# Attention, SoLU block and hard-swish block on one core: the second expert block as two sweeps of Strassen products, its activations in device memory between them

## The chip, the cores and the metric

One core of a Trainium2 chip. The time is that of the device in microseconds (us), median over runs; less is better.

## The reference

Chunked attention over 768 positions (4 batches, 8 heads, chunks of 32 with 16 before and 8 behind, and 8 memory rows), then two expert blocks over its 3072 tokens of 512 channels. The change touches the second:

```
def _moe_ref(x, w_in, w_out, g_ln):       # 3072x512, 512x1024, 1024x512
    h = x @ w_in
    ...
    solu = h * softmax(h)
    ...
    return (layer_norm(solu) * g_ln) @ w_out

def _moe2_ref(x, w_in, w_out):            # 3072x512, 512x2048, 2048x512
    h = x @ w_in
    relu6 = np.clip(h + 3.0, 0.0, 6.0)
    g = h * relu6 / 6.0
    return g @ w_out
```

All is float32. The kernel writes every operand of a large product as a high part in float32r (a cast) and a low part (operand less high part), and forms a product in three passes: high by high, high by low, low by high.

## The kernel before

The engines are programmed one by one, in the order in which the code stands; semaphores tie them together. `batch(b)` runs attention and the first expert block together, over eight steps `kk` per batch; `work` says which pieces fall into a step. `batch(B, last=True)` is the last one, with what is left: `turn_ln` (transposes of the normalised tile), `hidden` (first product) and `project` (second product, 24 matmuls of 384 tokens in each of four steps), whose result ACT copies in `store_x2` to `x2_out` and stores to device memory, `x2_scratch`. POOL's `normalise` makes the normalised tile.

The second block (`group`, six groups of 512 tokens) has all its weights in SBUF (`w2`, high and low). For each of 16 chunks of 128 hidden channels PE forms the hidden product (`hidden2`, through `split_products`, L505): 4 chunks of K by 3 passes, 12 matmuls of 512 tokens. ACT takes relu(h+3) (L753), DVE the minimum with 6 and the product with h (L896), ACT the high part (L763), DVE the low part (`low`, L783). Then `output` (L613): 4 token tiles by 3 passes, 12 matmuls of 512 output channels with `g_t` as weights. That is 6 x 16 x 12 = 1152 matmuls of each kind. Hidden products run two chunks ahead of output products. ACT's `copy_out` scales and copies the result (L745), SP stores it.

The weights of the second block come in 16 pieces: POOL issues two DMAs for each (L332, L337), ACT casts the high part (`high_weights`, L699), DVE subtracts the low part (`low_weights`). Five of them and the first tokens (`high_x2`, L687) fall into the last batch, where ACT and DVE have time, and so does the first hidden product, between the last transposes and the last four projections:

```
                    if w["mm2_3"]:
                        project(i, 3, ii, last and ii)
                    if last and kk == TPG:
                        hidden2(0, 0, 0, True)
```

## Time and profile before

| | |
|---|---|
| median of 3 runs | 984.63 us (984.3 to 985.13) |
| span of the profiled execution | 984.4 us |
| PE busy | 953.5 us, 97%, 5480 matmuls |
| weight loads of PE | 810.9 us, 82% |
| DVE / ACT / POOL busy | 484.9 / 410.6 / 101.3 us |
| bytes from and to device memory | 41.95 MB read, 12.58 MB written |
| mean granted clock of PE | 0.990 |

The profiled execution is given by its span, from its first to its last instruction; it lies 0.2 us under the median of the runs. PE means matmuls, PEld its weight loads, and a matmul's duration contains a pipeline's depth: the distance from one start to the next is its cost in a stream, not its duration. A busy share is an average over the whole program.

### The profile page before, as it was taken

The numbers are of one execution on the slowest core, as the hardware profiler recorded it, in microseconds if no ns is written. First come the engines' busy times: TensorE is split into PE (matmuls) and PEld (weight loads), VectorE is DVE, ScalarE is ACT, GpSimd is POOL, SyncE is SP. The second block draws the span as 40 slices with busy tenths as digits, with TensorE's granted clock in tenths as the row PEclk, the third lists the DMA queues.
The fourth block names the chain that finished last, engine by engine and source line by source line (L and its number), as shares of the span: only waits on it lengthen the run. The fifth ranks groups of instructions, "written<-read, shape, count | busy, mean of one in ns | idle before, by whom it ended". The sixth has DMA issues, their size and how long they took to land.

```text
span 984.4 us, 14941 instructions
## 1 busy us (share of the span) xinstructions
PE 953.5 (97%) x5480; PEld 810.9 (82%) x5480; DVE 484.9 (49%) x849; ACT 410.6 (42%) x1058; POOL 101.3 (10%) x138
## 2 busy tenths in 40 slices
PE   7788999999999999999999999999999999999998
PEld 6667888888888888899888888888878888888887
DVE  5787777777777767673652232223223322322221
ACT  5455565656555555543542322222223222323222
POOL 6363101001010101012310000000000000000000
PEclk9987999999999999999999999999999999999999
DMA  9533333332323432024430101001010101001001
GB/s 208 127 79 76 76 76 75 76 67 64 78 52 75 74 75 56 28 72 152 154 107 1 43 1 43 21 23 43 0 45 1 43 1 43 0 1 44 1 1 43
DMA packets 107304, 55.22 MB, mean 56 GB/s; under 512 B 93944, under 2 KB 98040, under 8 KB 107256
## 3 DMA queue, kind: packets, MB, share of 16 engines
q1 hardware_dynamic: 98904, 35.66, 16.0%
q0 software_dynamic: 3744, 12.59, 4.1%
q10 hardware_dynamic: 4608, 6.29, 1.8%
q8 instruction: 34, 0.56, 0.2%
q14 instruction: 14, 0.11, 0.0%
HBM read 41.95 MB, written 12.58 MB: 55 GB/s over the span
## 4 chain that ended last, share of the span: by engine, by line
PE 91%; DVE 5%; ACT 2%; issue 1%; DMA 1%; SPq 0%; DVEq 0%
PE banks L505 52%; PE banks L613 27%; PE banks L459 3%; PE banks L496 2%; PE banks L485 2%; PE banks L472 2%; PE banks L428 2%; DVE prob L807 1%; DMA k_in<-in_k_dram 1%; ACT prob L663 1%; DVE small L803 1%; PE banks L520 1%; DVE small L796 0%; DVE score L791 0%; DVE small L841 0%
## 5 line engine op out<-in xcount | busy, mean ns | idle before, releaser
L505 PE MATMUL banks<-x,w 128*128 128x512 f32 x1152 | 276.8, 389 | 0.7 <-issue 0.7
L613 PE MATMUL banks<-w,g_t 128*128 128x512 f32 x1152 | 276.4, 389 | 0.0
L505 PEld LDWEIGHTS banks<-x,w 128*128 128x128 f32 x1152 | 216.2, 188 | 45.7 <-issue 0.9
L613 PEld LDWEIGHTS banks<-w,g_t 128*128 128x128 f32 x1152 | 216.2, 188 | 45.1 <-DVE g_t L783 0.2
L896 DVE SCALAR_TENSOR_TENSOR g_raw<-g_raw,banks 128x512 f32<-128x512 f32 x96 | 66.1, 688 | 279.2 <-ACT g_raw L753 279.2
L753 ACT ACTIVATE g_raw<-banks,small 128x512 f32<-128x512 f32 x96 | 66.2, 690 | 275.0 <-PE banks L505 275.0
L505 PE MATMUL banks<-y_t,w_out 128*128 128x384 f32 x768 | 140.3, 337 | 0.0
L505 PE MATMUL banks<-w_in,x_t 128*128 128x512 f32 x552 | 133.7, 398 | 1.1 <-DVE solu L837 1.1
L505 PEld LDWEIGHTS banks<-y_t,w_out 128*128 128x128 f32 x768 | 132.1, 188 | 0.4
L505 PEld LDWEIGHTS banks<-w_in,x_t 128*128 128x128 f32 x552 | 103.5, 191 | 23.2 <-DVE solu L837 1.4
L663 ACT ACTIVATE prob<-score,small 96x128 f32<-96x128 f32 x256 | 99.2, 392 | 15.8 <-DVE small L796 15.8
L783 DVE TENSOR_TENSOR g_t<-g_raw,g_t 128x512 fp32r<-128x512 f32 x96 | 66.5, 693 | 70.5 <-ACT g_t L763 70.5
L763 ACT CAST g_t<-g_raw 128x512 fp32r<-128x512 f32 x96 | 59.7, 622 | 79.6 <-DVE g_raw L896 79.6
L791 DVE SCALAR_TENSOR_TENSOR score<-banks,mask 96x512 f32<-96x512 f32 x64 | 43.6, 681 | 27.0 <-PE banks L459 27.0
L807 DVE TENSOR_TENSOR prob<-prob,small 96x512 f32<-96x512 f32 x64 | 52.8, 825 | 2.2
L663 ACT ACTIVATION_READ_ACCUMULATOR prob<-score,small 96x1 f32 x256 | 48.7, 190 | 0.0
L392 POOL TENSOR_TENSOR small<-small 128x1 f32<-128x1 f32 x24 | 13.2, 552 | 339.7 <-DVE small L849 339.7
L796 DVE TENSOR_REDUCE small<-score 96x4 f32<-96x512 f32 x64 | 43.7, 682 | 2.2
L680 ACT COPY x_out<-banks 128x384 f32<-128x384 f32 x32 | 15.4, 480 | 67.8 <-PE banks L505 67.8
L669 ACT CAST x_t<-banks 128x384 fp32r<-128x384 f32 x32 | 15.3, 478 | 63.8 <-PE banks L485 63.8
L472 PE MATMUL banks<-ident,prob 96*128 96x96 f32 x256 | 30.5, 255 | 9.8 <-DVE prob L807 8.2
L459 PE MATMUL banks<-k_t,q_t 64*96 64x128 f32 x512 | 37.3, 287 | 1.1 <-ACT k_t L643 0.7
(61 smaller groups left out, 742.6 us busy)
## 6 DMA issues: line engine op xcount, KB each, us to landing
q_in<-in_q_dram SPq DMA_DIRECT2D x32, 192.0 KB, 3.7
x_scratch<-x_out ACTq DMA_DIRECT2D x32, 192.0 KB, 1.9
x_raw<-x_scratch SPq DMA_DIRECT2D x6, 1024.0 KB, 5.2
out_dram<-o_stage SPq DMA_DIRECT2D x24, 256.0 KB, 2.2
...
w_raw<-in_moe_w_in_dram POOLq DMA_DIRECT2D x16, 256.0 KB, 3.4
w_raw<-in_moe_w_out_dram POOLq DMA_DIRECT2D x16, 256.0 KB, 3.3
```

The lines of the kernel that those rows point to most:

```text
L459: mm = pe.matmul(score_ps[:, place(h), :], q_t[r, h // 2, :], k_t[r, h // 2, :], start=True, stop=True, skip_group_check=True)
L472: mm = pe.transpose(turn_ps[half][:, x * TQ:(x + 1) * TQ], prob[:, HB * half + x, :], ident[0:TQ, 0:TQ])
L505: mm = pe.matmul(psum, stationary(a, kc), moving(m, kc), start=(x == 0), stop=(x == len(passes) - 1))
L613: mm = pe.matmul(out_ps[t], g_t[:, c % 4, a, t * P:(t + 1) * P], w2[:, c, m, KD * P:PIECE], start=(c == 0 and x == 0), stop=(c == KF2 - 1 ...
L663: last = nc.scalar.activation(prob[:, h, :], score[:, h, :], ACT.Exp, bias=smax[:, h:h + 1], accum_out=ssum[:, h:h + 1])
L753: nc.scalar.activation(g_raw[:, c % 2, :], h2_ps[c % 4], ACT.Relu, bias=three).then_inc(relu_done, 1)
L763: nc.scalar.copy(g_t[:, c % 4, HI, :], g_raw[:, c % 2, :]).then_inc(g_hi_done, 1)
L783: return nc.vector.tensor_tensor(dst, src, hi.bitcast(F32), ALU.subtract)
L791: nc.vector.scalar_tensor_tensor(out=score[:, hs, :], in0=score_ps[:, hs, :], scalar=SCALE, in1=mask[:, kind, :].unsqueeze(1).broadcast_to ...
L796: nc.vector.tensor_reduce(smax[:, hs], score[:, hs, :], AX_X, ALU.max, negate=True).then_inc(smax_done, 1)
L807: nc.vector.tensor_tensor(prob[:, hs, :], prob[:, hs, :], srec[:, hs].unsqueeze(2).broadcast_to([TQ, HB, NK]), ALU.mult).then_inc(prob_don ...
L896: nc.vector.scalar_tensor_tensor(out=g_raw[:, c % 2, :], in0=g_raw[:, c % 2, :], scalar=6.0, in1=h2_ps[c % 4], op0=ALU.min, op1=ALU.mult). ...
```

## The change

Both products of the second block are split into 2 x 2 blocks and formed by Strassen's method in Winograd's form: seven products of blocks in place of eight, with four combinations of blocks on either operand ahead and seven additions behind. This needs all hidden channels before the second product, so there are two sweeps:

- First sweep: eight pairs `p` (hidden channel tiles p and p+8) by three units `g` of 1024 tokens. A unit is seven products of 2 chunks of K by 3 passes, 6 matmuls of 512 tokens each. POOL combines the weights (`mix_ws`) and subtracts their low parts (`low_ws`), ACT casts (`high_ws`). POOL combines x once (`mix_x`), ACT casts it (`high_xs`), DVE subtracts (`low_xs`); x stays in SBUF. ACT keeps partial sums (`keep`) and takes the relu (`relu_of`), DVE adds (`sum_of`) and gates (`gate`), SP stores the gated activations to `g_scratch` in device memory.
- Second sweep: six groups of 512 tokens by eight pairs `p`. SP loads four blocks of activations (`load_gs`), DVE combines (`mix_gs`, four operations of 256 columns), ACT casts 7 x 256 = 1792 columns (`high_gs`), DVE subtracts as many (`low_gs`), PE multiplies: 7 products x 2 x 3 = 42 matmuls of 256 columns. In the first group `mix_vs`, `high_vs` and `low_vs` (on POOL for odd, on DVE for even pairs) prepare the output weights. At a group's end ACT keeps the first product and DVE adds the others (`finish`).

The preparation of x and of the first weights goes into the last batch; `hidden2(0, 0)`, `high_x2` and `high_weights` are gone from it. The core of the diff:

```diff
@@ SP @@
+            load_ws(0)
+            sp.wait_ge(h_done, NG * MPG)
...
+            load_x(0)
+            sp.wait_ge(x2_done, KD * (NG - 1))
...
+            load_x(1)
+            sp.wait_ge(x2_done, KD * NG)
             for s in range(2):
                 sp.wait_ge(x2_free[s], 16 * (1 + 2 * NG))
-            load_x2(1)
...
+            load_x(2)
+            pair(0, first=True)
+            with sp.Fori(1, PAIRS - 1) as p:
+                pair(p)
+            pair(PAIRS - 1, last=True)
+            store_g(PAIRS - 1, 2, 12)
+            sp.wait_ge(prod_done[3], 3 * PAIRS)
+            for p in range(3, PAIRS):
+                load_vs(p)
@@ POOL @@
+            mix_ws(0)
+            low_ws(0)
+            mix_x(0)
+            mix_x(1)
+            mix_x(2)
+            mix_ws(1)
+            low_ws(1)
+            with pool.Fori(2, PAIRS) as p:
+                mix_ws(p)
+                low_ws(p)
+            for p in range(PAIRS):
+                mix_vs(p)
+                if p >= 2 and p % 2 == 0:
+                    low_vs(p - 1)
+            low_vs(PAIRS - 1)
@@ PE @@
-                    if last and kk == TPG:
-                        hidden2(0, 0, 0, True)
...
+            def product(i, g, ps, fresh):
+                passes = [(kc, a, m) for kc in range(2) for a, m in ((HI, HI), (HI, LO), (LO, HI))]
+                for x, (kc, a, m) in enumerate(passes):
+                    mm = pe.matmul(ps, ws[:, a, W_OF[i], kc, :], xs[g][X_OF[i]][:, m, kc, :],
+                                   start=(fresh and x == 0), stop=(x == len(passes) - 1), skip_group_check=True)
+                mm.then_inc(prod_done[i], 1)
...
+            def unit(p, g, first):
...
+                product(1, g, acc_ps[g], True)
+                if g > 0:
+                    third(p, g - 1, first)
...
+                pe.wait_ge(part_kept, 3 * u + 1)
+                product(6, g, acc_ps[g], False)
...
+                product(2, g, two_ps[g], True)
+                operands(7, p, g, first)
+                pe.wait_ge(part_kept, 3 * u + 2)
+                product(7, g, acc_ps[g], False)
...
+            def group(grp, first=False):
+                for p in range(PAIRS):
+                    pe.wait_ge(gs_lo_done, PAIRS * grp + p + 1)
...
+                    for i in M_ORDER:
+                        mm = mix_product(i, grp, p, first)
@@ ACT @@
                     if last and kk == 3:
-                        high_weights(0)
+                        act.wait_ge(wt_done, 4)
+                        high_ws(0, ORDER)
...
-                    if last and kk > 3:
-                        high_weights(kk - 3)
+                    if last and kk == 4:
+                        for n in range(7):
+                            high_xs(0, n)
+                    if last and kk in (5, 6):
+                        for n in range(4 * (kk - 5), 4 * (kk - 5) + 4 - (kk == 6)):
+                            high_xs(1, n)
...
+            for s in range(2):
+                act.wait_ge(x2_free[s], 16 * (1 + 2 * NG))
+            unit(0, 0, first=True)
+            high_xs(2, 0)
+            high_xs(2, 1)
+            unit(0, 1, first=True, then=[lambda n=n: high_xs(2, n) for n in range(2, 7)])
...
+            def group(grp, first=False, last=False):
+                for p in range(PAIRS):
+                    if first and p + 1 < PAIRS:
+                        high_vs(p + 1)
+                    if p + 2 < PAIRS:
+                        high_gs(grp, p + 2)
+                    elif not last:
+                        high_gs(grp + 1, p + 2 - PAIRS)
@@ DVE @@
+            def mix_gs(grp, p):
+                n = PAIRS * grp + p
+                x = p % 4
+                dve.wait_ge(g_here[x], 16 * (2 * grp + p // 4 + 1))
+                for k, (to, a, b, op) in enumerate(((4, 1, 3, ALU.add), (1, 0, 1, ALU.subtract),
+                                                    (5, 4, 0, ALU.subtract), (6, 2, 5, ALU.subtract))):
+                    if k:
+                        dve.wait_ge(gt_done, 4 * n + k)
+                    nc.vector.tensor_tensor(gs_raw[x][:, to, :], gs_raw[x][:, a, :], gs_raw[x][:, b, :], op
+                                            ).then_inc(gt_done, 1)
+
+            def low_gs(grp, p):
+                x = p % 4
+                dve.wait_ge(gs_hi_done, PAIRS * grp + p + 1)
+                low(gs[x][:, LO, :, :], gs_raw[x][:, :, :], gs[x][:, HI, :, :]).then_inc(gs_lo_done, 1)
...
+            def group(grp, first=False, last=False):
+                for p in range(PAIRS):
+                    if p + 2 < PAIRS:
+                        low_gs(grp, p + 2)
+                    elif not last:
+                        low_gs(grp + 1, p + 2 - PAIRS)
+                    if first and p + 1 < PAIRS and (p + 1) % 2 == 0:
+                        low_vs(p + 1)
+                    if p + 3 < PAIRS:
+                        mix_gs(grp, p + 3)
+                    elif not last:
+                        mix_gs(grp + 1, p + 3 - PAIRS)
+                finish(grp, first)
```

How the order moves, at three places. ACT in the last batch, before, from the last but one cast of a normalised tile (`y_t`) on; `x_out` is the copy of a projection, `w` a piece of weights:

```order
244 L656 CAST y_t_52<-banks 128x4x128 [waits y_turned] x2
245 L699 CAST w_69<-w_raw 128x1024 [waits w_raw_here0,h_done]
246 L680 COPY x_out<-banks 128x384 [waits x2_free1,x2_done]
247 L682 DMA x_scratch<-x_out 128x384 [waits x2_copied]
248 L656 CAST y_t_52<-banks 128x4x128 [waits y_turned] x2
249 L699 CAST w_69<-w_raw 128x1024 [waits w_raw_here1]
250 L680 COPY x_out<-banks 128x384 [waits x2_free0,x2_done]
251 L682 DMA x_scratch<-x_out 128x384 [waits x2_copied]
252 L699 CAST w_69<-w_raw 128x1024 [waits w_raw_here0]
253 L680 COPY x_out<-banks 128x384 [waits x2_free1,x2_done]
254 L682 DMA x_scratch<-x_out 128x384 [waits x2_copied]
255 L699 CAST w_69<-w_raw 128x1024 [waits w_raw_here1]
```

The same place now; `ws` are weights of the second block, `xs` its tokens:

```order
243 L885 CAST y_t_52<-banks 128x4x128 [waits y_turned] x2
244 L917 CAST ws<-ws_raw 128x256 [waits wt_done]
245 L917 CAST ws<-ws_raw 128x256 x6
246 L909 COPY x_out<-banks 128x384 [waits x2_free1,x2_done]
247 L911 DMA x_scratch<-x_out 128x384 [waits x2_copied]
248 L885 CAST y_t_52<-banks 128x4x128 [waits y_turned] x2
249 L926 CAST xs_0_70<-xs_raw_0_91 128x1024 [waits x_here0]
...
255 L926 CAST xs_2_72<-xs_raw_2_93 128x1024 [waits x_here0]
256 L909 COPY x_out<-banks 128x384 [waits x2_free0,x2_done]
257 L911 DMA x_scratch<-x_out 128x384 [waits x2_copied]
```

Between two copies of `x_out` stood one cast of a weight piece; now seven casts stand there, most of them with a wait for POOL's combinations (`xt_done`). What POOL does for them, behind its last normalisation (`ln`):

```order
98 L522 TENSOR_SCALAR ln<-solu,small 128x1024 [waits rstd_done,mask_ready]
99 L552 TENSOR_TENSOR ws_raw<-ws_raw 128x256 [waits ws_here]
100 L552 TENSOR_TENSOR ws_raw<-ws_raw 128x256 [waits wt_done] x3
101 L558 TENSOR_TENSOR ws<-ws_raw,ws 128x256 [waits ws_hi_done] x7
102 L567 TENSOR_TENSOR xs_raw_4_95<-xs_raw_6_97,xs_raw_0_91 128x1024 [waits x_here0]
```

Before, POOL issued weight DMAs at this place. DVE inside the loop of the second sweep, two steps of it (`gs` activations with high and low part, `gs_raw` as loaded and combined):

```order
497 L1088 TENSOR_TENSOR gs_125<-gs_raw_129,gs_125 128x1792 [waits gs_hi_done]
498 L1241 ISA
499 L1246 TENSOR_TENSOR gs_raw_126<-gs_raw_126 128x256 [waits g_here0]
500 L1245 ISA
501 L1246 TENSOR_TENSOR gs_raw_126<-gs_raw_126 128x256 [waits gt_done]
502 L1245 REGISTER_ALU
503 L1246 TENSOR_TENSOR gs_raw_126<-gs_raw_126 128x256 [waits gt_done]
504 L1245 REGISTER_ALU
505 L1246 TENSOR_TENSOR gs_raw_126<-gs_raw_126 128x256 [waits gt_done]
506 L1251 REGISTER_ALU
507 L1088 TENSOR_TENSOR gs_122<-gs_raw_126,gs_122 128x1792 [waits gs_hi_done]
508 L1246 TENSOR_TENSOR gs_raw_127<-gs_raw_127 128x256 [waits g_here1]
```

Before, the loop had an operation of 512 columns with a wait for `relu_done` and one with a wait for `g_hi_done`, 96 times; now four of 256 columns stand between two of 1792, each behind the one before it.

## Rows read from the trace of the kernel before

**Rows 1.** The page: busy time by engine, and the chain that ended last by engine
```profile
PE 953.5 (97%) x5480; PEld 810.9 (82%) x5480; DVE 484.9 (49%) x849; ACT 410.6 (42%) x1058; POOL 101.3 (10%) x138
...
PE 91%; DVE 5%; ACT 2%; issue 1%; DMA 1%; SPq 0%; DVEq 0%
```

**Rows 2.** By window: span; PE, PEld, DVE, ACT, POOL busy (count); PEclk, DMA, GB/s
```profile
25.00:34.00 9.00, 4.71 (x53) 3.80 (x52) 8.39 (x12) 4.59 (x20) 7.12 (x7) 1.00 0.88 193
34.10:37.30 3.20, 2.96 (x10) 2.48 (x11) 3.13 (x6) 1.98 (x9) 0.00 (x0) 0.50 0.46 169
...
760.00:980.00 220.00, 220.00 (x973) 182.21 (x972) 58.87 (x86) 60.23 (x96) 0.00 (x0) 1.00 0.04 15
```

**Rows 3.** Timeline of PE, 440 to 466: start, us, line, operation, shapes, count
```profile
440.22 1.03 PE L496 MATMUL banks<-ident,ln 128*128 128x128 f32 x8
441.01 2.99 PE L505 MATMUL banks<-x,w 128*128 128x512 f32 x12
443.84 16.83 PE L505 MATMUL banks<-y_t,w_out 128*128 128x384 f32 x96
460.51 5.64 PE L505 MATMUL banks<-x,w 128*128 128x512 f32 x24
```

**Rows 4.** DVE by line and shape: total busy, mean ns of one | idle before
```profile
L783 DVE TENSOR_TENSOR g_t<-g_raw,g_t 128x512 fp32r<-128x512 f32 x96 | 66.5, 693 | 70.5 <-ACT g_t L763 70.5
L896 DVE SCALAR_TENSOR_TENSOR g_raw<-g_raw,banks 128x512 f32<-128x512 f32 x96 | 66.1, 688 | 279.2 <-ACT g_raw L753 279.2
...
L783 DVE TENSOR_TENSOR w<-w_raw,w 128x1024 fp32r<-128x1024 f32 x16 | 20.4, 1272 | 20.5 <-ACT w L699 20.3
```

**Rows 5.** ACT by line and shape
```profile
L753 ACT ACTIVATE g_raw<-banks,small 128x512 f32<-128x512 f32 x96 | 66.2, 690 | 275.0 <-PE banks L505 275.0
L763 ACT CAST g_t<-g_raw 128x512 fp32r<-128x512 f32 x96 | 59.7, 622 | 79.6 <-DVE g_raw L896 79.6
...
L699 ACT CAST w<-w_raw 128x1024 fp32r<-128x1024 f32 x16 | 16.8, 1049 | 3.0 <-DMA w_raw<-in_moe_w_out_dram 1.8 <-ACT x_out L680 1.2
```

**Rows 6.** POOL by line and shape
```profile
L395 POOL TENSOR_SCALAR ln<-solu,small 128x1024 f32<-128x1024 f32 x24 | 28.8, 1200 | 4.3 <-POOL small L392 4.3
...
L358 POOL TENSOR_TENSOR w_out<-w_raw,w_out 128x1024 fp32r<-128x1024 f32 x4 | 9.7, 2433 | 0.3
...
L352 POOL TENSOR_SCALAR w_raw<-w_raw,small 128x512 f32<-128x512 f32 x8 | 5.4, 686 | 0.9 <-DMA w_raw<-in_moe_w_out_dram 0.9
```

**Rows 7.** DMA issues, the page's part 6
```profile
x_raw<-x_scratch SPq DMA_DIRECT2D x6, 1024.0 KB, 5.2
out_dram<-o_stage SPq DMA_DIRECT2D x24, 256.0 KB, 2.2
```

**Rows 8.** Weight loads of PE by line
```profile
L613 PEld LDWEIGHTS banks<-w,g_t 128*128 128x128 f32 x1152 | 216.2, 188 | 45.1 <-DVE g_t L783 0.2
```

**Rows 9.** Timelines of POOL (one row) and DVE (two rows), 30 to 34
```profile
30.39 2.34 POOL L358 TENSOR_TENSOR w_out<-w_raw,w_out 128x1024 fp32r<-128x1024 f32 x1
...
30.56 2.72 DVE L807 TENSOR_TENSOR prob<-prob,small 96x512 f32<-96x512 f32 x1
...
33.60 0.69 DVE L807 TENSOR_TENSOR prob<-prob,small 96x512 f32<-96x512 f32 x1
```

**Rows 10.** Timelines of ACT (two rows), DVE, POOL, 438 to 443
```profile
440.42 0.48 ACT L680 COPY x_out<-banks 128x384 f32<-128x384 f32 x1 [2.15 <-PE banks L505]
...
441.31 1.08 ACT L656 CAST y_t<-banks 128x512 fp32r<-128x512 f32 x2 [0.41 <-PE banks L496]
...
441.93 1.29 DVE L783 TENSOR_TENSOR y_t<-banks,y_t 128x512 fp32r<-128x512 f32 x2 [1.63 <-ACT y_t L656]
...
438.03 1.21 POOL L395 TENSOR_SCALAR ln<-solu,small 128x1024 f32<-128x1024 f32 x1 [0.18 <-POOL small L392]
```

**Rows 11.** Timelines of PE and of SP's queue at the end
```profile
972.92 8.32 PE L613 MATMUL banks<-w,g_t 128*128 128x512 f32 x36
...
979.86 2.37 SPq L296 DMA_DIRECT2D out_dram<-o_stage  x4
```

634 lines of the change are left out of this document (453 added, 181 removed).

## Prediction

> **What bounds the kernel now.** I read the page's busy times and its chain of waits first [rows 1]: TensorE (PE) is busy for 97% of the span, and 91% of the chain that ended last is PE. So time is won by fewer PE columns, as long as nobody else comes to set the pace. Next the stretches by window [rows 2]: in the 220 us from 760 on, PE issues 973 matmuls of 512 columns, one per 226.1 ns, at the full clock, while DVE is busy 27% and ACT 27%. The timeline of PE [rows 3] gives the other width: 96 matmuls of 384 columns between 443.84 and 460.51, one per 173.6 ns. Last the groups by shape for DVE, ACT and POOL [rows 4 to 6], since the change hands them much more.
>
> **Products, first sweep.** Eight products become seven at the same 512 columns: 8 x 3 x 7 x 6 = 1008 matmuls in place of 1152, that is 144 x 226.7 ns (226.1 rounded up for loop ends) = **32.6 us saved**. One unit (seven products of six matmuls) is 9.5 us. DVE has per unit seven operations of 0.69, 4.8 us, and ACT seven of 0.69 and a third of seven small casts, some 5.6 us [rows 4, 5]. Their chain also fits: product 3 of the unit before ends, DVE adds (0.69), ACT takes the relu (0.69) and keeps the partial sum (0.69 at most), 2.1 us with hand-offs, and product 7, which needs the last, starts 2.7 us after product 3 has ended. Stores of 256 KB take 2.2 us [rows 7] and have a whole unit. I cost this sweep at PE's own pace; if the casts of new weights fall into that chain, it loses some tenths in each of 16 units, at most 5 us.
>
> **Products, second sweep.** 6 x 8 x 7 x 6 = 2016 matmuls of 256 columns in place of 1152 of 512. No row has this form. A line through the two widths (0.41 ns per column) gives 121 ns; with 128 columns, transposes with the same 128-column weights follow each other at 0.79 us for 8, 99 ns [rows 3], so a weight load does not hold the stream above that there. From below I bound it at 113 (half of 226.1), from above at 188 ns, the length of one LDWEIGHTS [rows 8]. I take 121, the nearest in form: 42 matmuls, a pair of channel tiles, are **5.1 us**, the sweep 244 us, 17 under before, if PE sets the pace.
>
> **It does not: DVE and ACT do.** For each pair DVE forms four combinations of 256 columns, ACT casts 1792 columns, DVE subtracts 1792 columns. The program puts the subtraction for pair n directly behind the combinations of pair n and the combinations of n+1 behind it, so DVE stands idle during the cast, and the three times add up. DVE's tensor_tensor is 693 ns at 512 and 1272 at 1024 [rows 4], so 403 at 256 and 2140 at 1792; ACT's cast is 622 and 1049 [rows 5], so 1690 at 1792. 4 x 0.403 + 1.69 + 2.14 + 0.15 for hand-offs = **5.6 us per pair against PE's 5.1**. At the end of each group DVE adds seven products from PSUM at 0.69 (plus 0.03) = 5.0, behind which one cast (1.7) hides: 8 x 5.6 + 5.0 - 1.7 = **48.1 us per group** against 40.7 of PE. PE also waits at each group's start for the sums that free its banks, with gaps of some 4 us; it catches up within the group.
>
> **First group of that sweep.** DVE also subtracts three weight tiles (3 x 2.14), and POOL forms combinations and four subtractions. POOL's tensor_tensor takes 2.34 us at 1024, undisturbed [rows 9], 2.43 in the mean [rows 6]; with an intercept like that of its tensor_scalar (686 at 512, 1200 at 1024: 0.17) 0.72 at 256 and 4.0 at 1792. Five weight tiles are loaded only after the first sweep: 20 x 0.75 + 4 x 4.0 = 31 us. And POOL and DVE exclude each other: DVE's operation on prob from two SBUF operands starts at 30.56, inside POOL's from 30.39 to 32.73, and takes 2.72 in place of 0.69. I put the operations of ACT, DVE and POOL one behind the other, each engine in its order, POOL and DVE never at once. The subtractions of pairs 2 to 7 then end 9, 17, 31, 37, 51 and 56 us after the first sweep (two weight subtractions of 4.0 and 2.1 stand before every second one), those of the next group's pairs 0 and 1 at 67 and 73, the seven additions at 80, the next subtraction at **82**. With POOL free of charge the same list reads 7, 13, 20, 26, 34, 39, 47, 52, 59 and **61**. The Trainium skill, page "SBUF — State Buffer", section "Who interferes with whom", says that a DVE instruction with two SBUF inputs contends with a GpSimd one that reads SBUF, whoever came first holding the port. The trace agrees, with the 2.72 above; without that rule the first group would be 21 us shorter and the total 1016.
> After that four groups of 48.1 and five pairs of 5.6: 82 + 192.4 + 28 = 302.4, and PE's last pair with a lag of 2 us: **309.5 us from the end of the first sweep to PE's end**, where before had 1152 matmuls, 261.
>
> **Between the blocks.** Before, ACT's cast of a weight piece and 12 matmuls of the second block fill the last steps of the first block [rows 3, 10]. Now ACT casts seven pieces behind a wait for POOL's four combinations, and POOL comes to them only after its last normalisation, which ends at 439.24 [rows 10]. 439.3 + 3.2 = 442.5, casts 7 x 0.35 (0.41 by the same line, less what neighbours overlap) = 444.9, then the copy of x2 that stood at 440.42, and the cast of y_t, which began 0.9 us behind it and took 1.1: it now ends at 446.9, DVE's part 0.9 later, 447.8. PE has nothing after its transposes (440.22 and 0.8 to 0.9 us on, so 441.1): **6.7 us**. Four projections follow (4 x 4.2 = 16.8). The third needs the copy of the first, which in ACT's order stands behind seven casts that wait for POOL's combinations of x (4 x 2.4 at 1024 columns, some 10 us, and DVE's subtractions of 1.27 between them): first copy at 464 in place of 452, **8.5 us**. The fourth waits likewise for the next four casts: **6.2 us**. The first unit waits for ACT, which waits for the last store of x2: 2.3 us. The last third of x is loaded after that store: 2 MB, at 5.2 us per 1 MB [rows 7] 10.4 us, then POOL's combinations; meanwhile ACT stands before the casts in the second unit: 5.3 + 4.2 us. Sum **33.2 us**. After gaps the clock has fallen: at 34.10 to 37.30 it is 0.50 of full, the lower of the two levels, after a stretch in which PE was busy 4.71 of 9.00 us [rows 2], and 10 matmuls fill those 3.2 us; for five gaps I add 0 to 10, and take 4. **37 us** in all; what covers it, if POOL is quicker than I think, is nothing but its speed, so the range has 17 to 50.
> **Removed:** 16 casts and 16 subtractions of weights 24 of each for x, hidden behind PE now; POOL's 32 weight DMAs, hidden; both at nothing. What is added in DMA, 96 stores of 256 KB and 48 loads of 512 KB, is hidden as long as a load lands within the 10 us between its slot's release and its use.
>
> **The sum**, on the profiled execution (span 984.4; the median of runs is 984.63, 0.2 more): end of the first block 441.1 + 16.8 = 457.9; turn-over 37; first sweep 228.5; gives 723.4. Second sweep 309.5: 1032.9. Tail: before, PE ends at 981.24 and the last store at 984.4 [rows 11], 3.2; now an addition of 0.7 and a store of twice the size, 4.1. Total **1037 us**.
>
> **Rivals.** *PE sets the pace of the second sweep* (faster): if the cycle of combine, cast and subtract stays under 5.1 us, for which the wide operations would have to run 10% below the line through 512 and 1024 columns. Then 723.4 + 244 + 5 + 4 = 976, and about 950 with a light turn-over. For it stands only that DVE and ACT are at 27% now; against it the three durations. It decides at 5.1. *Weight loads bound the narrow matmuls* (slower still): 188 ns each, 2016 x 0.188 = 379, 723.4 + 379 + 8 = 1110. Against it the 99 ns of the transposes; for it, that those are another kind of matmul. The Trainium skill, "TensorE: Matmul & The Clock Gate", section "LDWEIGHTS (loading the stationary operand)", gives columns over 1.2, an estimate of 107 ns for 128 columns, by which the load would hide under 121; no run here shows that width. *POOL and DVE hardly collide and the turn-over is short*: 61 in place of 82 and 17 in place of 37: 996 to 1016; part of my range. *The gains and losses cancel*: total within 0.2%.
>
> **Chances.** The least difference that a measurement of this kernel tells from none is about 0.2%, 2 us. Forecast with its bounds (slower) 0.87; weight loads 0.05, slower too; PE's pace, faster, 0.06; cancelled 0.02. So slower 0.92, same 0.02, faster 0.06. Range: down by 20 for the first group, or by 20 for the turn-over, not both in full: 1003. Up by 13 for the turn-over, 10 for a cycle of 5.8 in place of 5.6 (44 times), 5 for the first sweep: 1065.
>
> **What would show it.** Right: granted clock lowered and gaps of PE between 441 and 510; units of 9.5 us after; DVE's 1792-column subtraction near 2.14 and ACT's cast near 1.69, taking turns; pairs at 5.6 and groups at 48; DVE operations of 4 us or more beside POOL in the first group. Wrong: matmuls of 256 columns above 130 ns apart; PE without idle time behind gs_lo_done; PE busy straight through 441 to 510.

## The result, and the profile after

The changed kernel took 1049.44 us (median of 4 runs, 1049.16 to 1051.67), the kernel before 984.46 beside it on the same chip (4 runs): ratio 1.0665, 95% interval 1.065 to 1.0681. The forecast of 1037 had the sign right, and the time lies in its range of 1003 to 1065. The profiled execution has a span of 1047.5 us, and the numbers below are set against that.

First the page of the changed kernel: busy time by engine; the chain that ended last, by engine; of the costliest groups those of the new block. They answer to [rows 1] and [rows 4, 5, 8].

```profile
PE 929.1 (89%) x6200; PEld 830.8 (79%) x6200; DVE 706.2 (67%) x1092; ACT 481.4 (46%) x1109; POOL 238.4 (23%) x242
...
PE 56%; DVE 19%; issue 8%; ACT 8%; POOL 5%; DMA 2%; SPq 1%; DVEq 0%; ACTq 0%; POOLq 0%
...
L841 PE MATMUL banks<-vs,gs 128*128 128x256 f32 x2016 | 260.3, 294 | 50.8 <-DVE vs L1088 21.8
L841 PEld LDWEIGHTS banks<-vs,gs 128*128 128x128 f32 x2016 | 257.7, 203 | 53.5 <-issue 39.6
L770 PE MATMUL banks<-xs,ws 128*128 128x512 f32 x1008 | 235.2, 395 | 18.5 <-ACT part L976 18.5
...
L1038 ACT CAST gs<-gs_raw 128x1792 fp32r<-128x1792 f32 x48 | 81.0, 1688 | 205.8 <-DVE gs_raw L1246 205.8
...
L1088 DVE TENSOR_TENSOR gs<-gs_raw,gs 128x1792 fp32r<-128x1792 f32 x48 | 101.3, 2110 | 75.9 <-ACT gs L1038 75.7
...
L1246 DVE TENSOR_TENSOR gs_raw<-gs_raw 128x256 f32<-128x256 f32 x192 | 90.9, 473 | 4.9
```

TensorE did less (929.1 us in place of 953.5) and the kernel took longer: PE's share of the chain went from 91% to 56%, and VectorE and ScalarE have 27% between them, where they had 7%. The idle time in the last columns says where: 50.8 us of PE in the second sweep and 18.5 in the first; and VectorE stood 75.7 us behind ScalarE's cast of the gates, while ScalarE stood 205.8 behind VectorE's combinations. These are two engines that wait for each other by turns.

Next the windows of the changed kernel (span; busy time and count of PE, PEld, DVE, ACT, POOL; PEclk; DMA; GB/s): a stretch between the blocks, the steady part of the first sweep, and 180 us of the second, beside [rows 2].

```profile
445.00:452.00 7.00, 5.31 (x17) 5.34 (x18) 3.95 (x3) 1.89 (x4) 6.84 (x6) 0.52 0.34 126
513.50:711.00 197.50, 197.49 (x870) 162.67 (x870) 101.58 (x146) 102.87 (x192) 59.16 (x72) 1.00 0.36 129
820.00:1000.00 180.00, 163.86 (x1298) 162.35 (x1296) 126.98 (x178) 54.29 (x35) 0.00 (x0) 0.94 0.35 111
```

The first sweep runs as forecast: 870 matmuls in 197.5 us, 227.0 ns each, no idle time. In the second, PE is idle 16 of 180 us while DVE is busy 71%. In the stretch behind a gap of 6.18 us the granted clock is about half (0.52), near the lower of the two levels, as in [rows 2].

The timeline of PE in the changed kernel (start, us, line, operation, count, idle time before) in its three troubled places: between the blocks, at the turn of the sweeps, and at the group starts.

```profile
446.69 10.88 PE L682 MATMUL banks<-y_t,w_out 128*128 128x384 f32 x48 [6.18 <-DVE y_t L1088]
461.88 6.02 PE L682 MATMUL banks<-y_t,w_out 128*128 128x384 f32 x24 [4.32 <-ACT x_out L909]
472.26 5.99 PE L682 MATMUL banks<-y_t,w_out 128*128 128x384 f32 x24 [4.36 <-ACT x_out L909]
...
513.51 8.68 PE L770 MATMUL banks<-xs,ws 128*128 128x512 f32 x37 [1.82 <-ACT part L976]
...
721.92 9.93 PE L770 MATMUL banks<-xs,ws 128*128 128x512 f32 x36 [10.69 <-ACT part L976]
731.69 5.20 PE L841 MATMUL banks<-vs,gs 128*128 128x256 f32 x42
746.99 7.51 PE L841 MATMUL banks<-vs,gs 128*128 128x256 f32 x42 [10.10 <-POOL vs L580]
758.93 11.82 PE L841 MATMUL banks<-vs,gs 128*128 128x256 f32 x84 [4.44 <-DVE vs L1088]
781.86 12.23 PE L841 MATMUL banks<-vs,gs 128*128 128x256 f32 x84 [11.11 <-DVE vs L1088]
800.31 12.34 PE L841 MATMUL banks<-vs,gs 128*128 128x256 f32 x90 [6.23 <-DVE vs L1088]
...
903.86 0.95 PE L841 MATMUL banks<-vs,gs 128*128 128x256 f32 x6 [1.68 <-ACT held L1077]
907.64 41.98 PE L841 MATMUL banks<-vs,gs 128*128 128x256 f32 x330 [2.83 <-DVE o_stage L1280]
```

With these rows the loss can be laid out. If PE had never waited, the changed kernel would read: end of the first block 457.3 (transposes end at 440.5, and 16.8 of projections), 1008 x 226.7 ns = 228.5, 2016 x 120.1 ns = 242.1, tail 4.7: **932.6 us**, 52 under the span before. It took 115 more:

| stretch | lost by PE, us | from |
|---|---|---|
| between the blocks, up to 513.51 | 33 | 513.51 less 102 matmuls of the block (23.1), less 457.3 |
| turn of the sweeps | 12.4 | gap 10.69, and 36 matmuls in 9.93 in place of 8.2 |
| first group of the second sweep | 39.7 | 80.1 (731.7 to 811.8, the start of the next group's first matmul) in place of 336 x 120.1 ns = 40.4 |
| its five other groups | 29.2 | 231.0 (811.8 to 1042.8) in place of 201.8 |

The cycle of the steady groups, in the timeline of VectorE and then of ScalarE of the changed kernel:

```profile
803.63 2.03 DVE L1088 TENSOR_TENSOR gs<-gs_raw,gs 128x1792 fp32r<-128x1792 f32 x1 [1.75 <-ACT gs L1038]
805.58 1.80 DVE L1246 TENSOR_TENSOR gs_raw<-gs_raw 128x256 f32<-128x256 f32 x4
809.13 2.03 DVE L1088 TENSOR_TENSOR gs<-gs_raw,gs 128x1792 fp32r<-128x1792 f32 x1 [1.76 <-ACT gs L1038]
```

```profile
807.41 1.69 ACT L1038 CAST gs<-gs_raw 128x1792 fp32r<-128x1792 f32 x1 [3.81 <-DVE gs_raw L1246]
```

Subtraction 2.03, combinations 1.80, idle 1.76 while ScalarE casts for 1.69: from 803.63 to 809.13 is 5.50 us. PE's six-by-seven matmuls need 5.04. Of 47.0 us per group VectorE spends seven such cycles and 8.5 us on the last one, which has the additions in it; in that time it waits for nothing but ScalarE's cast. PE runs six of the eight pairs of a group at 5.04 us each, has then caught up, and pays at the group's start: gaps of 1.7 and 2.8 us, and a stretch at half clock behind them (granted clock 0.50 from 907.6 to 911).

### The profile page after: what moved, and what is told of

Its sections match the earlier page's. It is cut to its first block, busy times and chain, and to the rows that moved or that the text cites. A ratio compares the mean times of both kernels' runs of the same rounds, so it can differ in the third digit from the quotient of the medians.

```text
span 1047.5 us, 17721 instructions
## 1 busy us (share of the span) xinstructions
PE 929.1 (89%) x6200; PEld 830.8 (79%) x6200; DVE 706.2 (67%) x1092; ACT 481.4 (46%) x1109; POOL 238.4 (23%) x242
## 4 chain that ended last, share of the span: by engine, by line
PE 56%; DVE 19%; issue 8%; ACT 8%; POOL 5%; DMA 2%; SPq 1%; DVEq 0%; ACTq 0%; POOLq 0%
PE banks L682 22%; PE banks L770 19%; DVE gs_raw L1246 7%; ACT gs L1038 6%; PE banks L841 4%; POOL xs_raw L567 3%; PE banks L636 3%; DVE gs L1088 3%; PE banks L662 2%; PE banks L673 2%; PE banks L649 2%; PE banks L605 2%; DVE vs L1088 2%; DVE held L1280 1%; DVE prob L1112 1%
## 5 line engine op out<-in xcount | busy, mean ns | idle before, releaser
L841 PE MATMUL banks<-vs,gs 128*128 128x256 f32 x2016 | 260.3, 294 | 50.8 <-DVE vs L1088 21.8
L841 PEld LDWEIGHTS banks<-vs,gs 128*128 128x128 f32 x2016 | 257.7, 203 | 53.5 <-issue 39.6
L770 PE MATMUL banks<-xs,ws 128*128 128x512 f32 x1008 | 235.2, 395 | 18.5 <-ACT part L976 18.5
L770 PEld LDWEIGHTS banks<-xs,ws 128*128 128x128 f32 x1008 | 191.4, 191 | 62.1 <-ACT part L976 11.1
L1038 ACT CAST gs<-gs_raw 128x1792 fp32r<-128x1792 f32 x48 | 81.0, 1688 | 205.8 <-DVE gs_raw L1246 205.8
L682 PE MATMUL banks<-y_t,w_out 128*128 128x384 f32 x768 | 146.4, 347 | 14.9 <-ACT x_out L909 8.7
L1088 DVE TENSOR_TENSOR gs<-gs_raw,gs 128x1792 fp32r<-128x1792 f32 x48 | 101.3, 2110 | 75.9 <-ACT gs L1038 75.7
L682 PEld LDWEIGHTS banks<-w_in,x_t 128*128 128x128 f32 x552 | 103.2, 190 | 23.1 <-DVE solu L1142 1.4
L992 ACT ACTIVATE relu<-part,small 128x512 f32<-128x512 f32 x72 | 52.2, 724 | 97.4 <-DVE part L1203 97.4
L1246 DVE TENSOR_TENSOR gs_raw<-gs_raw 128x256 f32<-128x256 f32 x192 | 90.9, 473 | 4.9
L1212 DVE SCALAR_TENSOR_TENSOR part<-relu,part 128x512 f32<-128x512 f32 x72 | 54.0, 750 | 52.8 <-ACT relu L992 52.8
L1203 DVE TENSOR_TENSOR part<-part,banks 128x512 f32<-128x512 f32 x72 | 49.5, 687 | 53.0 <-PE banks L770 52.8
L976 ACT COPY part<-banks 128x512 f32<-128x512 f32 x72 | 41.6, 578 | 15.9 <-PE banks L770 13.5
```

What stands on the lines that cost most here:

```text
L682: mm = pe.matmul(psum, stationary(a, kc), moving(m, kc), start=(x == 0), stop=(x == len(passes) - 1))
L770: mm = pe.matmul(ps, ws[:, a, W_OF[i], kc, :], xs[g][X_OF[i]][:, m, kc, :], start=(fresh and x == 0), stop=(x == len(passes) - 1), skip_gr ...
L841: mm = pe.matmul(m_ps[i][:, s, :], gs[x][:, a, G_OF[i], s * P:(s + 1) * P], vs[p][:, m, V_OF[i], :], start=(p == 0 and s == 0 and n == 0), ...
L992: nc.scalar.activation(relu[r][:, :], src, ACT.Relu, bias=three).then_inc(relu_done[kind], 1)
L1038: nc.scalar.copy(gs[p % 4][:, HI, :, :], gs_raw[p % 4][:, :, :]).then_inc(gs_hi_done, 1)
L1088: return nc.vector.tensor_tensor(dst, src, hi.bitcast(F32), ALU.subtract)
```

## The experiments

Each run is set beside the kernel before on its own chip (984.3 to 985.3 us in median), and beside the 1047.5 of span that the change has.

### dve_ahead: the combination ahead of the subtraction

```diff
                 for p in range(PAIRS):
+                    if p + 3 < PAIRS:
+                        mix_gs(grp, p + 3)
+                    elif not last:
+                        mix_gs(grp + 1, p + 3 - PAIRS)
                     if p + 2 < PAIRS:
                         low_gs(grp, p + 2)
...
-                    if p + 3 < PAIRS:
-                        mix_gs(grp, p + 3)
-                    elif not last:
-                        mix_gs(grp + 1, p + 3 - PAIRS)
```

> The same instructions, with DVE's combinations for pair p+3 ahead of its subtraction for pair p+2 (they stood behind it), all through the second sweep. Theory 1 (combinations, cast and subtraction follow each other in one cycle, because DVE waits through ACT's cast): the cast now runs beside DVE's next combinations, DVE needs 3.8 us per pair, PE's 42 matmuls at 120 ns set the pace with 5.04 us. At a group's end the additions still come late by some 4 us, so groups of about 44 in place of 47.8 us; with the first and the last group about 22 us less, 1027. Theory 2 (DVE's total work, or the landing of the activations from device memory, sets the pace): nothing changes, 1049, groups of 47.8.

Measured: 1042.76 us (1039.34 to 1044.95), ratio 1.0572 (1.0547 to 1.0597). The timeline of PE in this run at a group start, and that of VectorE ahead of it:

```profile
907.39 42.08 PE L841 MATMUL banks<-vs,gs 128*128 128x256 f32 x336 [2.67 <-DVE o_stage L1280]
```

```profile
903.00 1.80 DVE L1246 TENSOR_TENSOR gs_raw<-gs_raw 128x256 f32<-128x256 f32 x4 [1.11 <-DMA gs_raw<-g_scratch]
904.72 2.02 DVE L1088 TENSOR_TENSOR gs<-gs_raw,gs 128x1792 fp32r<-128x1792 f32 x1
```

The wait for the cast is gone, and VectorE waits for loads of gates instead, which start when PE has freed a slot: within a group PE sets the pace now. A group takes 45.0 us ((997.08 - 817.01) / 4, by PE's gaps) in place of 47.0. What is left is not the cycle but the group's end: a gap of 2.7 us, and matmuls at a lower clock behind it (granted clock 0.76 from 907 to 914). So the cause was right and its price a third of what I expected, 6.7 us in place of 22. The second sweep alone is 7.1 us shorter in the profiled executions (304.0 in place of 311.1).

### dve_ahead_sums: the sums one step earlier as well

On top of that, the last combination of a group moved behind `finish`, so that the sums stand ahead of it:

```diff
-                    elif not last:
+                    elif not last and p < PAIRS - 1:
                         mix_gs(grp + 1, p + 3 - PAIRS)
...
                 finish(grp, first)
+                if not last:
+                    mix_gs(grp + 1, 2)
```

> As dve_ahead, and at a group's end the seven additions come ahead of the combinations for pair 2 of the next group, whose activations land only when PE has used its buffer. Theory 1: PE's wait at the start of a group shrinks from about 4 us to about 1, groups of about 41.5 us, total about 1014. Theory 2: nothing changes against after (1049). A mixed case: the time of dve_ahead, if PE's wait at the group's start comes from the subtraction and not from the additions.

Measured: 1021.89 us (1020.19 to 1023.16), ratio 1.0366 (1.0348 to 1.0384). PE's timeline of this run:

```profile
897.94 40.57 PE L841 MATMUL banks<-vs,gs 128*128 128x256 f32 x336 [0.22 <-DVE held L1280]
938.69 40.58 PE L841 MATMUL banks<-vs,gs 128*128 128x256 f32 x336 [0.18 <-DVE held L1280]
```

A group takes 40.8 us, 4.2 less again, at PE's own pace. The five groups take 203.7 us in place of 231.0, so 27.3 of the 29.2 us that they lost come from the order of one engine's instructions. No operation became shorter and none was left out: in the second sweep VectorE's subtractions of gates last 2203 ns in the mean (2112 in the change) and its combinations 481 (475). The sums' move alone was not run, so how the two moves share the gain is known in this order only. The 256-column matmuls take 120.7 ns over a whole group, against 120.1 in an undisturbed stretch, with a weight load for each, so the loads hide under them.

### pool_write_only: does GpSimd's reading hold VectorE?

```diff
-                nc.gpsimd.tensor_tensor(vs[p][:, LO, :, :], vs_raw[p][:, :, :], vs[p][:, HI, :, :].bitcast(F32),
-                                        ALU.subtract).then_inc(vs_lo_odd, 1)
+                nc.gpsimd.memset(vs[p][:, LO, :, :].bitcast(F32), 0.0).then_inc(vs_lo_odd, 1)
```

> POOL's four subtractions of 1792 columns of output weights (low parts of odd pairs) become memsets of the same columns to zero: the low parts of the weights of pairs 1, 3, 5 and 7 are left out. POOL writes as much but reads nothing. Theory 1 (POOL and DVE exclude each other where both read SBUF): DVE's subtractions of 1792 columns that took 5.8 us beside POOL's take 2.0 beside a memset, the first group is some 8 to 12 us shorter, total about 1039. Theory 2 (any operation of POOL holds DVE off): those subtractions take about 2.0 plus the memset's length, 3.7 us, and the total is about 1043.

Measured: 1035.91 us (1034.66 to 1038.2), ratio 1.0514 (1.0491 to 1.0537). This kernel leaves the low parts of the odd pairs' weights out. The rows of the changed kernel, GpSimd's and then VectorE's:

```profile
775.63 4.21 POOL L580 TENSOR_TENSOR vs<-vs_raw,vs 128x1792 fp32r<-128x1792 f32 x1 [4.58 <-ACT vs L1042]
```

```profile
775.94 5.78 DVE L1088 TENSOR_TENSOR vs<-vs_raw,vs 128x1792 fp32r<-128x1792 f32 x1
```

and those of this run, in the same order:

```profile
768.78 1.59 POOL L580 MEMSET vs<- 128x1792 f32 x1 [5.02 <-ACT vs L1041]
```

```profile
769.11 2.02 DVE L1087 TENSOR_TENSOR vs<-vs_raw,vs 128x1792 fp32r<-128x1792 f32 x1
...
771.04 3.56 DVE L1245 TENSOR_TENSOR gs_raw<-gs_raw 128x256 f32<-128x256 f32 x4
```

Beside a subtraction of GpSimd that reads two SBUF operands, VectorE's row lasts 5.78 us, from 0.31 behind GpSimd's start to 1.88 behind its end: in length that is GpSimd's instruction waited out and then VectorE's own 2.02. Beside a GpSimd operation that writes as much and reads nothing, it lasts 2.02. GpSimd's combinations, which still read, go on stretching VectorE's (3.56 for four in place of 1.80). That is the rule which the prediction drew from the Trainium skill, page "SBUF — State Buffer", section "Who interferes with whom"; the same section excepts a GpSimd instruction that only writes, and this run shows that too. The time fell by 12.4 us in span and 13.5 in median. In the changed kernel three of VectorE's rows stand beside GpSimd's subtractions (5.78, 5.78 and 5.57 in place of 2.02), 11 us of stretch. Together with those beside GpSimd's combinations, VectorE's rows of the first group are 20.8 us longer than at 2.02 and 0.45 each, which is the size that the forecast gave to this collision (21). The total does not price the collision alone: GpSimd's own rows fell from 4 us or more to 1.59 as well, four times, and its next combinations start sooner for it.

### last_unit: preparation inside the last unit of the first sweep

```diff
-            high_vs(0)
-            high_gs(0, 0)
-            unit(last, 2)
+            unit(last, 2, then=[lambda: None, lambda: None, lambda: high_vs(0), lambda: None,
+                                lambda: high_gs(0, 0)])
...
-            low_vs(0)
             mix_gs(0, 0)
-            unit(last, 2, then=[lambda: mix_gs(0, 1), lambda: low_gs(0, 0)])
+            unit(last, 2, then=[lambda: mix_gs(0, 1), lambda: low_vs(0), lambda: None, lambda: low_gs(0, 0)])
```

> ACT's casts of the first output weights and the first activations, and DVE's subtraction of those weights, stand inside the last unit of the first sweep, ahead of which they stood; nothing else is changed. Theory 1 (PE's gap from 711 to 722 is ACT waiting for POOL's and DVE's preparation of the second sweep, in its queue ahead of the copy that PE needs): the gap goes, at most 3 us of it come back at the start of the second sweep, and a stretch at half clock goes too: about 1040. Theory 2 (the weights of the second sweep land late anyway, and PE waits for them then): the gap moves behind the last unit, total 1047 to 1049.

Measured: 1044.97 us (1042.44 to 1046.84), ratio 1.061 (1.0582 to 1.0637). ScalarE's timeline of the changed kernel, where the 10.69 comes from:

```profile
714.21 1.68 ACT L1042 CAST vs<-vs_raw 128x1792 fp32r<-128x1792 f32 x1 [4.96 <-POOL vs_raw L575]
719.70 1.69 ACT L1038 CAST gs<-gs_raw 128x1792 fp32r<-128x1792 f32 x1 [3.81 <-DVE gs_raw L1246]
721.29 0.58 ACT L976 COPY part<-banks 128x512 f32<-128x512 f32 x1
```

and PE's of this run:

```profile
717.74 7.35 PE L770 MATMUL banks<-xs,ws 128*128 128x512 f32 x24 [2.87 <-ACT part L976]
726.55 5.30 PE L841 MATMUL banks<-vs,gs 128*128 128x256 f32 x42 [1.46 <-DVE gs L1087]
740.69 4.61 PE L841 MATMUL banks<-vs,gs 128*128 128x256 f32 x20 [8.84 <-POOL vs L580]
```

and GpSimd's of this run:

```profile
728.25 8.36 POOL L575 TENSOR_TENSOR vs_raw<-vs_raw 128x256 f32<-128x256 f32 x8 [13.14 <-DMA vs_raw<-in_moe_w_out_dram]
```

ScalarE stood 4.96 us for GpSimd's combinations and 3.81 for VectorE's with a copy behind them that PE needed. With the casts behind that copy, the gap falls from 10.69 to 2.87, one of 1.46 appears ahead of the second sweep, and that sweep starts at 726.55, 5.1 us sooner. The run as a whole gained 4.5, half of the 9 expected: the place is shown, but not all of the gap goes. The first group behind it keeps its length (79.0 us in place of 80.1): GpSimd's combinations for pairs 1 and 2 start at 728.25 in place of 735.92, and PE still waits 8.84 us for the first of them.

### stores_first, x_on_dve, casts_between_stores: the way between the blocks

Three kernels on the 33 us ahead of 513.51. In the profiled executions of the change and of the four kernels so far, which have the same code up to there, that instant lies between 512.65 and 514.94, so differences under some 2 us say nothing. The first kernel puts the casts of `ws` behind those of y_t, all casts of the first third of `xs` behind the last store of x2, and those of the second third, with VectorE's subtractions, into the first unit:

```diff
-                    if last and kk == 3:
-                        act.wait_ge(wt_done, 4)
-                        high_ws(0, ORDER)
                     if last and kk == 4:
-                        for n in range(7):
-                            high_xs(0, n)
-                    if last and kk in (5, 6):
-                        for n in range(4 * (kk - 5), 4 * (kk - 5) + 4 - (kk == 6)):
-                            high_xs(1, n)
+                        act.wait_ge(wt_done, 4)
+                        high_ws(0, ORDER)
...
             act.wait_ge(three_ready, 1)
+            for n in range(7):
+                high_xs(0, n)
...
+            unit(0, 0, first=True, then=[lambda n=n: high_xs(1, n) for n in range(7)])
+            high_xs(1, 6)
```

> Turn-over between the blocks: ACT's seven casts of the first weights move behind the last casts of the normalised tile, and all casts of x behind the last copy of a projection, so that no copy stands behind a cast that waits for POOL; DVE's subtractions follow. Amounts of work are unchanged. Theory 1 (PE's gaps between 440 and 478 are ACT's queue: copies behind casts that wait for POOL's combinations): the gap of 6.2 us before the projections shrinks to about 1.7, those of 4.3 and 4.4 between them go, the last third of x is loaded some 18 us earlier, and the total falls by about 17 us to about 1032. Theory 2 (POOL's combinations are the bound of this stretch, wherever the casts stand): the gaps move to the first units, total about 1045.

Measured: 1048.42 us (1046.77 to 1050.2), ratio 1.0643 (1.0619 to 1.0668). PE's timeline of this run:

```profile
442.30 16.91 PE L682 MATMUL banks<-y_t,w_out 128*128 128x384 f32 x96 [2.11 <-DVE y_t L1085]
462.64 2.90 PE L770 MATMUL banks<-xs,ws 128*128 128x512 f32 x6 [3.43 <-DVE xs L1085]
...
483.11 7.11 PE L770 MATMUL banks<-xs,ws 128*128 128x512 f32 x18 [7.75 <-ACT part L970]
```

The four projections run without a gap, as expected: PE's first three gaps shrink from 14.9 us to 2.1. But PE is steady from 508.71, only 4.8 us sooner, and the total is not clear of the change's: a miss of 16 us. ScalarE's queue was where PE waited, but the work behind it bounded the stretch. VectorE's row of this run, and GpSimd's in the changed kernel:

```profile
461.27 18.93 DVE L1085 TENSOR_TENSOR xs<-xs_raw,xs 128x1024 fp32r<-128x1024 f32 x7 [19.12 <-ACT xs L926]
```

```profile
446.88 23.82 POOL L567 TENSOR_TENSOR xs_raw<-xs_raw,xs_raw 128x1024 f32<-128x1024 f32 x8
```

With the casts behind the stores VectorE stood idle for 19.12 us, and then its seven subtractions took 2.7 us each beside GpSimd's combinations, where one alone takes 1.22; PE's gaps of 3.43 and 7.75 stand behind them.

The second leaves ScalarE's order as the change has it and moves `mix_x` from GpSimd to VectorE, ahead of the subtractions that read it (its definition, on VectorE with the same four operations, is left out here):

```diff
-            mix_x(0)
-            mix_x(1)
-            mix_x(2)
...
                 i = ORDER[n]
+                if n == 0:
+                    mix_x(g)
```

> The twelve combinations of x (1024 columns each) move from POOL to DVE, directly ahead of DVE's subtractions for the same tokens; ACT's order is as in after. Theory 1 (they are slow on POOL, 2.35 us against 1.27, and POOL and DVE hold each other off): first copy behind the casts at about 455 in place of 461, second at about 467 in place of 472, all that follows about 6 us earlier and a combination time of 5 in place of 11 us for the last third: total about 1037. Theory 2 (ACT's order alone makes the gaps): 1045 or more.

Measured: 1041.92 us (1041.0 to 1047.61), ratio 1.0594 (1.0556 to 1.0631); PE is steady from 506.38, 7.1 sooner. The third has that, puts the casts of `ws` later as `stores_first` did, and spreads ScalarE's casts of x three by three between the stores of x2:

```diff
+                    if last and kk == 7:
+                        for n in range(3):
+                            high_xs(1, n)
...
                     if last and kk == 4:
-                        for n in range(7):
+                        act.wait_ge(wt_done, 4)
+                        high_ws(0, ORDER)
+                        high_xs(0, 0)
+                    if last and kk in (5, 6):
+                        for n in range(3 * (kk - 5) + 1, 3 * (kk - 5) + 4):
                             high_xs(0, n)
-                    if last and kk in (5, 6):
-                        for n in range(4 * (kk - 5), 4 * (kk - 5) + 4 - (kk == 6)):
-                            high_xs(1, n)
...
+            unit(0, 0, first=True, then=[lambda n=n: high_xs(1, n) for n in range(3, 7)])
```

> Both of the last two: combinations of x on DVE, and ACT's casts of x spread three by three between the copies of the projections, those of the second third partly inside the first unit. Theory 1: projections run without gaps from about 442 to 459, the first unit starts at about 460 in place of 478, total about 1024. If one of the two theories of the turn-over is wrong, it is no better than the better of the two runs alone.

Measured: 1039.97 us (1035.93 to 1042.06), ratio 1.0547 (1.0514 to 1.058); steady from 502.13, 11.4 sooner than in the change, 8.9 of which reach the second sweep. So two causes are there: GpSimd's combinations of x, and ScalarE's order. `x_on_dve` does not part GpSimd's slowness (2.34 us at this width [rows 9] where VectorE takes 1.22) from its collision with VectorE. The second cause shows in PE's steady start (4.3 us sooner again) and not in the total, where the two kernels' times overlap. Taking both away gives 11 of 33 us. What is left is work on VectorE (it is busy 19.0 of the 21 us from 480 to 501 in the kernel `all`) and, ahead of PE's first gap there, ScalarE's waits for VectorE's combinations (3.73) and for the last store of x2 to land (2.04).

### all, all_2, all_sp: can the change be made to pay?

`all` joins casts_between_stores, last_unit and dve_ahead_sums, and gives the four subtractions of output weights that GpSimd did to VectorE (PE's wait for them changes with it):

```diff
                 mix_vs(p)
-                if p >= 2 and p % 2 == 0:
-                    low_vs(p - 1)
-            low_vs(PAIRS - 1)
...
-                    if first and p + 1 < PAIRS and (p + 1) % 2 == 0:
+                    if first and p + 1 < PAIRS:
                         low_vs(p + 1)
```

> All changes together: casts between stores with x on DVE, the last unit's order, DVE's combinations ahead of its subtractions with the additions ahead of the next group's third combination, and POOL's four subtractions of output weights moved to DVE (2.0 in place of 4.0 us of a port that only one of them holds). If the gains of the parts add up (25, 4 to 6, 27 and about 7 us): 1049 - 65 = 984, the time of before. The first group of the second sweep keeps it from less: its combinations, casts and subtractions of output weights take DVE and POOL some 65 us where PE needs 40.

Measured: 995.22 us (994.68 to 995.96), ratio 1.0104 (1.0086 to 1.0123), 54 us under the change, 11 over the 984 of the expectation and still 1.0% over the kernel before. PE's timeline of this run:

```profile
483.45 4.56 PE L764 MATMUL banks<-xs,ws 128*128 128x512 f32 x12 [5.08 <-ACT part L969]
...
728.77 6.95 PE L835 MATMUL banks<-vs,gs 128*128 128x256 f32 x42 [10.05 <-DVE vs L1080]
739.52 6.72 PE L835 MATMUL banks<-vs,gs 128*128 128x256 f32 x42 [3.80 <-DVE vs L1080]
...
773.07 55.94 PE L835 MATMUL banks<-vs,gs 128*128 128x256 f32 x450 [4.85 <-DVE vs L1080]
```

What is left is the way between the blocks, 20.8 us (501.19 less 23.1 and 457.3), and the first group, 71.5 us in place of 40.4 (from 713.42 to the first matmul of the next group at 784.93). Two more kernels went for those gaps. `all_2` moves ScalarE's last store of x2 ahead of the casts of the second third of x, one cast behind a part copy (left out here), and three loads, two of weights and one of gates, ahead of the stores in the last unit:

```diff
-                    if last and kk == 7:
-                        for n in range(3):
-                            high_xs(1, n)
                     if w["mm2_3"]:
                         store_x2(i, 3, last and ii)
+                    if last and kk == 7:
+                        high_xs(1, 0)
...
+                    if last and g == 2:
+                        sp.wait_ge(prod_done[3], 3 * p + 2)
+                        load_vs(1)
+                        load_gs(0, 3)
+                        load_vs(2)
                     if not (first and g == 0):
                         store_g(*before_unit(p, g), 12)
...
-                    if last and g == 2:
-                        sp.wait_ge(prod_done[3], 3 * p + 2)
-                        load_gs(0, 3)
-                        load_vs(1)
-                        load_vs(2)
```

> The kernel of the run all, with three moves more. (1) ScalarE: the last copy of x_out and its store come ahead of the casts of the second projection, which go behind it and between the part copies of the unit (0, 0); the gap of 5.30 us at 466.45 in that run stood behind a store that was issued at 463.71, after a cast that waited for VectorE. Theory: the gap falls to some 2 us. (2) ScalarE: the second cast of the third projection stands behind the first part copy of the unit (0, 1), where it stood ahead of it and waited for VectorE; the gap of 5.08 at 483.45 falls to under 1. (3) SyncE: in the last unit of the first sweep the loads of the output weights of pairs 1 and 2 and of pair 3's gates are issued ahead of the stores of the gates, not behind the first two of them; GpSimd's combination at 715.38, which waited for that load, comes some 5 us earlier, and the gap of 10.05 at 728.77 falls by 3 to 5. Sum: 995.2 - 3.3 - 4.5 - 4 = 983 us, about the kernel before (985.0, ratio 0.998). Rival: the preparation is bound by the sums of VectorE's work, as in stores_first, and the gaps only move: 990 to 995. A reading over 990 speaks for the rival.

Measured: 997.93 us (997.4 to 998.54), ratio 1.0135 (1.0118 to 1.0152), above the rival's 990 to 995 too. Against `all` it is 2.7 us slower, on another chip, and the intervals of the two ratios touch: it gained nothing, and may have lost. The gap of 5.30 fell to 1.90 and came back as 6.83 at 488.05; the gap of 10.05 fell to 5.58 and the next one rose from 3.80 to 7.04, and the first group takes 73.0 us in place of 71.5. `all_sp` takes only the loads, and lets the five last weight tiles take turns with the gates (the loads in the last unit, moved as in `all_2`, are left out here, and so is the shift of the group's own loads to pair 7 and later):

```diff
             pair(PAIRS - 1, last=True)
+            sp.wait_ge(prod_done[3], 3 * PAIRS)
+            load_vs(3)
             store_g(PAIRS - 1, 2, 12)
-            sp.wait_ge(prod_done[3], 3 * PAIRS)
-            for p in range(3, PAIRS):
-                load_vs(p)
+            load_vs(4)
+            for p in range(4, PAIRS - 1):
+                sp.wait_ge(gs_used, p - 3)
+                load_gs(0, p)
+                load_vs(p + 1)
```

> The kernel of the run all with SyncE's loads around the turn of the sweeps in another order, and nothing of all_2's ScalarE moves. The output weights of pairs 1 and 2 are issued ahead of the stores in the last unit of the first sweep; the five last weight tiles, which stood as one block of 2.5 MB ahead of the gates of pair 4, now take turns with the gates of pairs 4 to 6. In all, VectorE waited 2.60, 0.30, 2.25 and 0.97 us for gates in the first group, and GpSimd's weights of pair 1 came at 715.38. Theory (late loads are the rest of the first group's loss beside VectorE's own work): the gap of 10.05 falls to about 5.6, as in all_2, and those four waits fall by about 4 in sum: 995.2 - 4.5 - 4 = 987 us, ratio 1.002. Rival (VectorE's work sets the first group, 5.9 us per pair against TensorE's 5.1, and loads that come earlier only move the gaps): 993 to 996, with VectorE busy nearly without idle time between 713 and 773.

Measured: 1000.5 us (998.53 to 1002.28), ratio 1.0157 (1.0142 to 1.0173). VectorE's timeline of this run:

```profile
758.04 1.80 DVE L1252 TENSOR_TENSOR gs_raw<-gs_raw 128x256 f32<-128x256 f32 x4 [4.67 <-DMA gs_raw<-g_scratch]
...
775.50 1.81 DVE L1252 TENSOR_TENSOR gs_raw<-gs_raw 128x256 f32<-128x256 f32 x4 [6.20 <-DMA gs_raw<-g_scratch]
```

Counted in the order of the program, VectorE's combinations for pairs 4, 5, 6 and 7 and for the next group's first two waited 0, 2.44, 0.18, 4.67, 0 and 6.20 us for gates, where they waited 2.60, 0.30, 2.25, 0.97, 4.44 and 0 in `all`: 13.5 in sum in place of 10.6 (the expectation has the first four of these). From pair 4 on a load of gates starts only when PE has freed its slot, in both kernels, so loads that are issued in another order move the waits and do not take them away. The gap of 10.05 fell to 8.04 and not to 5.6, and the first group takes 75.6 us. Neither side of the expectation holds: the time is above both, and VectorE was busy 48.3 of the 60 us from 713 on, not nearly all of them.

The rows of `all` hint at a third reading. VectorE's timeline ahead of PE's gap of 4.85:

```profile
767.25 1.80 DVE L1248 TENSOR_TENSOR gs_raw<-gs_raw 128x256 f32<-128x256 f32 x4 [4.44 <-DMA gs_raw<-g_scratch]
...
770.90 2.02 DVE L1080 TENSOR_TENSOR vs<-vs_raw,vs 128x1792 fp32r<-128x1792 f32 x1
```

The subtraction of weights for which PE stands idle (it ends at 772.92, PE starts at 773.07) is queued behind a combination that waits 4.44 us for gates, whose slot PE has to free: in the first group the new order has a wait of its own. No run takes it away there alone. So whether the rest of the first group's loss is late loads, VectorE's 5.9 us per pair or this order stays open, and no version run here beats the kernel before.

## Why the prediction was right, step by step

- *Products, first sweep*, 226.7 ns each: 227.0 in the window. Right: over 870 matmuls the casts of new weights cost 0.3 us at most.
- *Products, second sweep*, 121 ns with weight loads hidden: 120.1 within a run of matmuls and 120.7 over a PE-bound group, though a LDWEIGHTS row lasts 203 ns in the mean. The weight-load rival is out. What the Trainium skill gives in "TensorE: Matmul & The Clock Gate", section "LDWEIGHTS (loading the stationary operand)", 107 ns by estimate, fits under that; the row's 203 ns is then not the cost of a load in a stream.
- *It does not: DVE and ACT do*: 4 x 0.45 + 1.69 + 2.03 = 5.5 per pair where I had 5.6, groups of 47.0 where I had 48.1. Two errors offset each other in it: the combinations take 0.45 each where I had 0.403, the subtraction 2.03 where I had 2.14. ScalarE's line through two widths hit its 1792-column cast within 2 ns (1690 against 1688); VectorE's gave 2140 against 2030 undisturbed. That the three add up is shown by `dve_ahead`, which ends the adding up. PE does catch up within a group, as I wrote, so VectorE's cycle, with ScalarE's cast in it, sets the 47.0. What I did not see is that the group's end is a second limit just below it: with the cycle undone, PE's wait for the sums and the lower clock behind it still cost 4 us per group.
- *First group*: additions ended at 80 us in the forecast. They end 86 us after the sweep's start in the trace (817.7 less 731.7), and PE's first group lasts 80.1. The mechanism was right, as `pool_write_only` shows, and its size too (20.8 us of stretch in VectorE's rows for my 21). In the trace the lateness is there from pair 2 on, behind a wait of GpSimd for the weights of pairs 1 and 2, which my list had there at the start. GpSimd's timeline of the changed kernel, and that of SyncE's queue:

```profile
735.92 7.00 POOL L575 TENSOR_TENSOR vs_raw<-vs_raw 128x256 f32<-128x256 f32 x8 [21.74 <-DMA vs_raw<-in_moe_w_out_dram]
```

```profile
723.24 6.65 SPq L358 DMA_DIRECT2D g_scratch<-part  x2
...
730.41 1.01 SPq L370 DMA_DIRECT2D vs_raw<-in_moe_w_out_dram  x2
```

  The loads stand behind stores of the last unit. `all_2` and `all_sp` issued them sooner, on top of other edits, and gained nothing in sum, and in `last_unit` the weights came 7.7 us sooner and the first group kept its length; alone this was not tried.
- *Between the blocks*: 33.1 against 37, and part of that agreement is luck. PE's idle rows up to 513.51 sum to 22.7 us where I had 33.2, with the first three at 6.2, 4.3 and 4.4 in place of 6.7, 8.5 and 6.2; the other 10.4 us are matmuls at the lower clock, for which I had taken 4. GpSimd's combinations of x took 2.98, not 2.4, beside VectorE, but the copies of x2 came at 461.36 and 471.74 where I had 464 and, by my own terms, 475.
- *The step that failed* is a term that I put at nothing: the turn of the sweeps. I put 457.9 + 37 + 228.5 = 723.4 for the start of the second sweep and left out that ScalarE's program has two casts for the second sweep ahead of the last unit of the first, each behind another engine. It cost 12.4 us, and 731.7 is 8 above my number for that alone (less 4 from the term before). The time is in the range all the same because the range was wide enough for a term of 12 that nobody had in it.
- The sum of the errors: +8.3 to the second sweep's start, +1.6 in it (first group +6, groups -4), +0.6 in the tail: 10.5, from 1037.0 to 1047.5.
